# Scattering routed rows to their experts' slots during the layers, and reading them with plain transfers in the expert steps

## The reference, cut to what matters

```python
# attention between 512 tokens x 64 and 32 states x 64, per batch (8) and head (8), both ways
attn_out = concat([softmax(x state^T) state, softmax(state x^T) x], axis=2)   # 544 rows a batch
x = attn_out.transpose(0, 2, 1, 3).reshape(4608, 512)
y = leaky(x @ w_in) @ w_out                     # 512 -> 2048 -> 512, a dense layer
e_idx = argmax(y @ w_gate); gate = softmax(y @ w_gate)[e_idx]
eom = sigmoid(y @ w_output_gate)                # 8 experts, one for each row
for e in range(8):
    out[mask] = gate * eom[:, e] * (relu(y[mask] @ w1[e]) @ w2[e])   # 512 -> 1024 -> 512
```

## Time and profile before

| | us |
|---|---|
| median of 3 runs | 1158.89 (1156.09 to 1159.37) |
| the profiled execution | 1158.76 |
| its span | 1157.0 |
| PE busy in the span | 1114.1 |
| DVE, ACT, POOL busy | 632.6, 405.8, 275.6 |

### The profile page before, as it was taken

The page is one execution under the profiler, slowest core; times in us unless marked ns, Lnnn a source line. Parts: engine busy times, 40 slices in busy tenths (PEclk is TensorE's granted clock), DMA queues, the critical chain, the costliest instruction groups (busy, mean ns, idle before and its releaser), DMA issues.

```text
span 1157.0 us, 18341 instructions
## 1 busy us (share of the span) xinstructions
PE 1114.1 (96%) x6530; PEld 903.9 (78%) x6531; DVE 632.6 (55%) x1421; ACT 405.8 (35%) x754; POOL 275.6 (24%) x337
## 2 busy tenths in 40 slices
PE   5999999999999999999999999999999999888995
PEld 2777777777777777777777888889899989678884
DVE  6684574764854746747554577553433436366342
ACT  4344334434433443344343553321211214244211
POOL 1000001010010010000100203554455365655643
PEclk8999999999999999999999999999999999999998
DMA  9311120120210201200102411761111124443211
GB/s 346 125 45 37 37 78 1 42 73 1 76 40 18 80 19 37 79 1 1 37 1 75 126 38 48 201 195 55 39 48 59 37 56 98 144 105 107 55 39 35
DMA packets 41054, 79.01 MB, mean 68 GB/s; under 512 B 11398, under 2 KB 13190, under 8 KB 40967
## 3 DMA queue, kind: packets, MB, share of 16 engines
q1 hardware_dynamic: 29957, 53.48, 15.2%
q0 software_dynamic: 11040, 24.77, 7.5%
HBM read 60.31 MB, written 20.61 MB: 70 GB/s over the span
## 4 chain that ended last, share of the span: by engine, by line
PE 80%; DVE 6%; issue 4%; DMA 4%; POOL 2%; ACT 1%; POOLq 1%; SPq 0%; DVEq 0%; ACTq 0%
PE bank L529 25%; PE bank L531 24%; PE bank L530 24%; PE bank L562 3%; DMA raw<-w_dram 2%; POOL xq L438 2%; DMA xq<-rows_dram,part_now 2%; PE bank L580 1%; PE bank L596 1%; DVE w_lo L1338 1%; PE bank L604 1%; PE bank L540 1%; PE bank L569 1%; DVE g_buf L1213 0%; DVE o_buf L1600 0%
## 5 line engine op out<-in xcount | busy, mean ns | idle before, releaser
L529 PE MATMUL bank<-wout_lo,gT_hi 128*128 128x512 f32 x544 | 216.0, 397 | 0.0
L531 PE MATMUL bank<-wout_hi,gT_hi 128*128 128x512 f32 x544 | 212.7, 391 | 0.0
L530 PE MATMUL bank<-wout_hi,gT_lo 128*128 128x512 f32 x544 | 212.2, 390 | 0.0
L438 POOL DMA_INDIRECT xq<-rows_dram,part_now x160 | 170.5, 1066 | 69.4 <-issue 54.7
L423 POOL DMA_INDIRECT slots_dram<-tok_i,pos_i x34 | 34.4, 1010 | 616.3 <-DVE pos_i L1313 608.6
L1213 DVE TENSOR_TENSOR g_buf<-g_buf,bank 128x512 f32<-128x512 f32 (+1 forms) x144 | 94.3, 655 | 107.2 <-ACT g_buf L963 106.9
L529 PE MATMUL bank<-xgT_lo,w_hi 128*128 128x256 f32 x512 | 146.3, 286 | 6.0 <-DVE hT_lo L1469 4.7
L530 PE MATMUL bank<-xgT_hi,w_lo 128*128 128x256 f32 x512 | 145.6, 284 | 0.0
L531 PE MATMUL bank<-xgT_hi,w_hi 128*128 128x256 f32 x512 | 145.5, 284 | 0.0
L963 ACT ACTIVATE g_buf<-bank 128x512 f32<-128x512 f32 (+1 forms) x144 | 82.5, 573 | 151.7 <-PE bank L531 150.2
L1217 DVE TENSOR_TENSOR gT_lo<-g_buf,gT_hi 128x512 fp32r<-128x512 f32 (+1 forms) x144 | 95.4, 662 | 72.9 <-ACT gT_hi L969 71.4
(11 more groups left out here) (227 smaller groups left out, 1764.0 us busy)
## 6 DMA issues: line engine op xcount, KB each, us to landing
raw<-w_dram SPq DMA_DIRECT2D x20, 512.0 KB, 8.9
raw<-w_dram SPq DMA_DIRECT2D x10, 1024.0 KB, 14.5
rows_dram<-y_buf SPq DMA_DIRECT2D x8, 1032.0 KB, 4.5
X<-x_in_dram SPq DMA_DIRECT2D x8, 1024.0 KB, 5.5
XT<-xT_in_dram SPq DMA_DIRECT2D x7, 1024.0 KB, 5.7
win<-w_in_dram SPq DMA_DIRECT2D x4, 1024.0 KB, 11.6
y_buf<-w_out_dram POOLq DMA_DIRECT2D x6, 512.0 KB, 7.2
xq<-rows_dram,part_now POOLq DMA_INDIRECT x160
```

Source lines behind the costliest of these rows:

```text
L438: pool.indirect_dma_start(out=xq[:, 4 * u + a, :], out_offset=None, in_=quarters_dram, in_offset=bass.IndirectOffsetOnAxis(ap=part_now[:, ...
L529: pe.matmul(o, l_hi, r_lo, start=first, stop=False)
L530: pe.matmul(o, l_lo, r_hi, start=False, stop=False)
L531: return pe.matmul(o, l_hi, r_hi, start=False, stop=last)
```

## The change

It does this:

- `rows_dram` becomes a table in the order of slots: 8 experts x 4608 slots of 516 floats. `store_rows` goes. In each layer DVE works out a row's slot at f = 12 (`route_rows`), and POOL scatters the 512 rows with four indirect DMAs (`set_rows`) ahead of `set_slots`. `keep_y` waits for them (`rows_set`).
- In layer B the splits of the first expert's first pieces move from f = 8, 10 to 11, 13; gates and ranks from 11 to 8, rows to 9, slots to 10; and the first step's rows are transposed by DVE at f = 14 and split before the layer's last copies.
- A step's rows come with `load_rows`: four plain DMAs of 32 partitions x 8 x 512 bytes and one of 128 x 2 x 8 bytes for the scales, on POOL's queue. `part_row`, `order_rows`, `flip_rows` and the copies of row numbers go.
- Slots behind an expert's last row have to hold finite numbers. SP copies 4.2 MB from `x_in` to slots 256 to 511 of each expert near the start (0.45 MB before, for another purpose), and `fill_tails` writes 256 slots behind each expert's last row from SBUF: eight indirect DMAs of 128 x 4128 bytes, 4.2 MB, and a ninth of at most eight rows. POOL may load the rows of the third and all later steps (those for `turn_quarters(2)` on) only when `filled` shows all nine to have landed.
- `turn_quarters(i + 1)` moves to behind the fifth `h_lo` of a full step and to the front of a half step; PE's first `down` tile waits for each of the last three `h_lo` by itself.
- SP loads the next `w1` as soon as four pieces are split, `w2` after eight.
- The routing of the state rows moves into the first step's `up`.

```diff
-FIRST_PIECE_AT = {0: 2, 3: 3, 8: 0, 10: 1}
+FIRST_PIECE_AT = {0: 2, 3: 3, 11: 0, 13: 1}
-    rows_dram = nc.dram_tensor("rows_dram", (NT, ROW), fp32).ap()
+    rows_dram = nc.dram_tensor("rows_dram", (SLOTS, ROW), fp32).ap()
...
+            sp.dma_start(rows_dram.rearrange("(e s) n -> e s n", e=E)[:, PAIR:2 * PAIR, :],
+                         x_in.rearrange("b s n -> (b s n)")[0:E * PAIR * ROW].rearrange("(e s n) -> e s n", e=E, s=PAIR)).then_inc(slots_clear, 16)
...
-                if b >= 1:
-                    store_rows(b - 1)
...
             sp.wait_ge(ctl_ready, 1)
-            sp.wait_ge(gathered, 64)
+            sp.wait_ge(rows_in, 160)
...
+                    sp.wait_ge(e_lo_done, w1_splits)
+                    load_w1(expert)
                     sp.wait_ge(e_lo_done, splits)
-                    load_expert(expert, between)
+                    load_w2(expert)
-            load_planned(1, between=192)
+            load_planned(1)
...
+            def set_rows(blocks, tiles):
+                pool.wait_ge(slots_clear, 32)
+                pool.wait_ge(row_ready, blocks)
+                for t in range(tiles):
+                    pool.indirect_dma_start(out=rows_dram, out_offset=bass.IndirectOffsetOnAxis(ap=row_i[:, t:t + 1], axis=0),
+                                            in_=y_buf[:, t, :], in_offset=None,
+                                            bounds_check=SLOTS - 1, oob_is_err=False).then_inc(rows_set, 16)
+            def load_rows(col):
+                two = rows_by_tile[bass.ds(col, 2), :, :]
+                for q in range(DC):
+                    pool.dma_start(xq[NS * q:NS * q + NS, :, :],
+                                   two[:, :, QW * q:QW * q + P].rearrange("u (a t) n -> t (u a) n", t=NS)).then_inc(rows_in, 16)
+                pool.dma_start(s_in[:, :, :], two[:, :, P:P + 2].rearrange("u p o -> p u o")).then_inc(rows_in, 16)
+            def fill_tails():
+                pool.wait_ge(rows_set, 64 * B + 32)
+                pool.wait_ge(fill_ready, 1)
+                some_rows = w1_hi[0][:, :, :].bitcast(fp32).rearrange("p k f -> p (k f)")
+                for e in range(E):
+                    pool.indirect_dma_start(out=rows_dram.rearrange("(a two) n -> a (two n)", two=2),
+                                            out_offset=bass.IndirectOffsetOnAxis(ap=fill_i[:, e:e + 1], axis=0),
+                                            in_=some_rows[:, 0:2 * ROW], in_offset=None,
+                                            bounds_check=SLOTS // 2 - 1, oob_is_err=False).then_inc(filled, 16)
...
             with pool.Fori(1, B) as blocks:
+                set_rows(blocks, 4)
                 set_slots(blocks, 4)
+            pool.wait_ge(rows_set, 64 * (B - 1))
+            load_rows(first_col)
+            set_rows(B, 4)
+            set_slots(B, 4)
+            set_rows(B + 1, 2)
+            set_slots(B + 1, 2)
...
+            pool.wait_ge(s_taken, 2)
+            pool.wait_ge(rows_set, 64 * B + 32)
+            load_rows(second_col)
+            fill_tails()
...
+                        pool.wait_ge(filled, 16 * E + 16)
                         pool.wait_ge(s_taken, n)
-                        pool.tensor_copy(part_now[:, :, :], part_row[:, :, bass.ds(col, 2)]).then_inc(rows_copied, 1)
-                        gather_step(n, n)
+                        load_rows(col)
...
-                late = F2 - 1 if tiles == 2 else F2 // 2
+                at_once = 5 if tiles == 2 else F2 // 2
...
+                        elif u == 0 and f >= at_once and tiles == 2:
+                            pe.wait_ge(h_lo_done, F2 * i + f + 1)
...
+            def turn_quarters(i):
+                dve.wait_ge(rows_in, 80 * i + 80)
...
+                    if b == B and f == 14:
+                        dve.wait_ge(y_kept_a, 2 * B)
+                        dve.wait_ge(rows_set, 64 * B)
+                        turn_quarters(0)
...
+            fill_rows()
             plan_order()
...
             plan_steps()
             dve.wait_ge(s_taken, 2)
             dve.tensor_copy(s_now[:, :], s_next[:, :]).then_inc(s_moved, 1)
+            turn_quarters(1)
...
                 if tiles == 2:
-                    for f in range(F2):
+                    for f in range(5):
                         h_lo(i, f)
                     turn_quarters(i + 1)
+                    for f in range(5, F2):
+                        h_lo(i, f)
                 else:
+                    turn_quarters(i + 1)
                     h_lo_turned(i, 0)
-                    turn_quarters(i + 1)
                     h_lo_turned(i, 1)
```

More of the change, by code:

```diff
@@ L425, in set_slots @@
                                             bounds_check=P * COLS - 1, oob_is_err=False).then_inc(slots_set, 16)
[L427 to L440, removed]
@@ L511, in _ @@
             total, after, after2 = load_ctl(pool, 8, MAXP), load_ctl(pool, 25, MAXP + 1), load_ctl(pool, 26, MAXP + 2)
-            all_gathered = load_ctl(pool, 44, 128 * MAXP, 1)
-            gather_step(total, after)
+            all_loaded = load_ctl(pool, 44, 80 * MAXP + 80, 1)
+            pool.wait_ge(filled, 16 * E + 16)
+            pool.wait_ge(s_taken, after)
+            load_rows(first_col)
             next_tokens(after)
@@ L750, in beside_down @@
                     make_v(b, 3)
-                elif f == 11 and r is not None:
+                elif f == (11 if b < B else 8) and r is not None:
                     if b < B:
@@ L791, in _ @@
                 layer(b)
-            def flip_rows(i, halves=(0, 1)):
-                pe.wait_ge(rows_ordered, 2 * i + 2)
-                for n in halves:
-                    for c in (2 * n, 2 * n + 1):
-                        for u in range(2):
-                            o = PAIR * (c % 2) + P * u
-                            last = pe.transpose(t_b[n][:, o:o + P], xr[:, u, c, :], ident)
-                    last.then_inc(t_ready, 1)
             def rows_wait(i, k):
@@ L876, in first_step_and_last_routing @@
                     for k in range(DC):
+                        if f == 0:
+                            rows_wait(0, k)
+                        elif f == 3 and k == 2:
+                            ranks(B, 2, rank_bank=oacc[0])
                         last = product(h_b[f % 4][:, 0:PAIR], w1_hi[0][:, k, fs], w1_lo[0][:, k, fs], xgT_hi[:, k, :], xgT_lo[:, k, :],
@@ L1316, in route_slots @@
                     step(dve.tensor_scalar(tokf[:, 0:T], tokf[:, 0:T], float(S + NS), None, ALU.add))
-                    step.end()
+                step.end()
             w8_row = const[0:1, C_W8:C_W8 + E]
@@ L1346, in states_lo, with rows_lo @@
                 dve.tensor_tensor(sr_lo[:, :, :], sread[:, :, :], sr_hi[:, :, :].bitcast(fp32), ALU.subtract).then_inc(sr_lo_done, 1)
+            def rows_lo(i):
+                for n in range(2):
+                    dve.wait_ge(xg_hi_done, 2 * i + n + 1)
+                    dve.tensor_tensor(xgT_lo[:, 2 * n:2 * n + 2, :], t_b[n][:, :].rearrange("p (c t) -> p c t", c=2),
+                                      xgT_hi[:, 2 * n:2 * n + 2, :].bitcast(fp32), ALU.subtract).then_inc(xg_lo_done, 1)
+            def turn_quarters(i):
+                dve.wait_ge(rows_in, 80 * i + 80)
+                for n in range(2):
+                    dve.transpose(t_b[n][:, :].rearrange("p (k g t) -> p g k t", k=2, t=NS),
+                                  xq[:, :, 2 * NS * n:2 * NS * n + 2 * NS].rearrange("p g (k d) -> p g k d", k=2)).then_inc(t_ready, 1)
+                if not (isinstance(i, int) and i == 0):
+                    dve.wait_ge(s_moved, i)
+                dve.wait_ge(t_ready, 2 * i + 2)
+                dve.tensor_copy(s_next[:, :].rearrange("p (u o) -> p u o", o=1), s_in[:, :, 0:1]).then_inc(s_taken, 2 if isinstance(i, int) and i == 0 else 1)
             def layer(b):
@@ L1419, in _ @@
             dve.memset(ones[:, :], 1.0).then_inc(ones_ready, 1)
-            for q in range(4):
-                dve.memset(quarter[NS * q:NS * q + NS, :], float(q))
             for half in range(2):
```

263 lines of the change are left out of this document (109 added, 154 removed).

## The result

The changed kernel takes 1164.19 us (median of 5 runs, 1162.5 to 1164.8) where the kernel before took 1158.4 beside it: ratio 1.0052, 95% interval 1.0036 to 1.0068. It is slower by 5.8 us; the forecast had 1158.3. The profiled execution took 1162.5 us, its span 1160.9, 3.9 more than before.

The account below looks back on a forecast made before the run. PE bounds the kernel, busy 1114.1 of 1157.0 us. 1158.76 + 9.2 (second step) - 9.7 (half steps and switches) = 1158.3 us; range 1150.5 to 1165.5, likeliest case (gain and loss cancel, 0.38) 1155 to 1162.

Parts of the forecast that it names:

- Layers: Layers before the expert phase: added POOL scatters stay hidden, change taken as 0, upper bound 1 us.
- First step: First expert step: starts at 699.2 without flips and gather wait, second step at 727.0 instead of 729.7; gain not counted.
- Second step: Second expert step: PE idles 11 us at `down`'s sixth block for rows loaded behind the fills; net +9.2 us.
- the clock behind the long wait: Second expert step: slower PE clock after the 11 us idle, costing 1.7 us.
- The starved queue: Second step: weights' burst holds back POOL's fills, landing about 744.5; rival starved to the weights' end: 1163, chance 0.04.
- Half steps and switches: Small experts' five steps: gather waits and late-weight wait go, a split wait of 3.0 comes; 86.6 against 96.3, -9.7 us.
- the 1.6 of clock that was given an even chance: Small experts: slow clock after the 3.0 split wait, 1.6 us at even chance, counted as 0.8.
- the two clock terms named at the start: Small experts before the change: slow PE clock at 1056 to 1059.4 and in step 1005 to 1023, some 3.5 us together.
- the load's "11 us": Half steps: trigger 2.8 us in (5.7 for a new expert), 4.5 issue, 2.5 landing; rows ready before `turn_quarters` at 13.6.
- rival 2: Row loads on POOL's queue no quicker than gathers, 13 us to landing: +6 second step, +2 half steps, 1166; chance 0.22.
- Rival 1: Second step: queues share evenly, fills land at 740.5, PE goes on at 750; 1155, or down to 1150; chance 0.36.
- Rival 3: Second step: wait at `filled` hidden because DVE reaches `turn_quarters(2)` late, after 751; part of rival 1's chance.

Follow-up runs that it names:

- late_w1: Changed kernel with 32 unused bytes ahead of `phase`, but both next-expert weights again wait for all eight splits; 1.0027 of the kernel before.
- after_plus32: Changed kernel with an unused 32-byte tile ahead of `phase`, restoring the earlier SBUF offsets from `XT` on; 0.9906 of the kernel before.
- after_plus32_b: Changed kernel with 32 unused bytes ahead of `phase`, repeated on another chip; 0.9917 of the kernel before.

## Why the prediction was wrong

- **Layers, "I take 0, upper bound 1 us": the step that failed.** Measured +5.4 up to the first step, and +1.5 in the full steps, which were taken as equal ("22.4 before and after"). It looked for waits that the scatters could cause, and PE's waits there came to only 0.2 us more in all (4.0 for 3.8). It did not look at what the diff does to the addresses of tiles it doesn't mention. Shown by moving the tiles alone, in both kernels. Which of the tiles matters, and what in SBUF makes the difference, was not tried.
- **First step.** Forecast 27.8 us from its first product to that of the second step (699.2 to 727.0), measured 28.5. Right within 0.7.
- **Second step.** Right in kind: one wait for the sixth block of `hT_lo`, from the loads behind the fills. Forecast +9.2 up to the third step's end, +9.0 counted from the first step's start, measured +7.0. Counted from that start, the fills landed at 42.8 us (45.3 forecast), PE went on at 52.2 (54.2). So of the idle time, 5.9 for 11.3, 2.0 are rows that came earlier, and 3.4 are no gain but a slower PE: it came to the sixth block at 46.3 (42.9 forecast). The forecast had priced the clock behind the long wait only, at 1.7 us (from rows 4, where it names rows 6), which is about what it cost there. The 2.85 us of idling at the step's start cost clock too, and more, because PE had work through the whole slow stretch:

```profile
732.00:739.50 7.50, 6.62 (x32) 6.62 (x33) 0.88 (x3) 0.77 (x2) 4.04 (x9) 0.54 0.98 325
752.50:760.00 7.50, 3.37 (x9) 2.71 (x10) 5.27 (x10) 4.53 (x6) 3.78 (x5) 0.54 0.40 121
```

  0.54 is the 1.2 GHz level nearly throughout. In the first window PE works at it from 732.88 to 738.9: 28 products of 256 columns at 0.213 us each instead of 0.119, 2.6 us. In the second it works at it only from 756.63 to 759.5: seven products of 512 columns, 1.4 us. The starved queue was wrong: both queues moved. The rule of the Trainium skill ("DMA: Bandwidth & Descriptors", the section on queues, rings and completion order) that a DMA engine goes round robin between its queues fits 737 to 743, 325 of the profile's packets to 300. In 743 to 747 it was 568 to 151; the rows do not tell whether POOL's queue still had work on every engine then, so they neither bear the rule out nor refute it.
- **Half steps and switches.** -9.7 forecast, -8.6 measured, and -9.3 with the layout undone (87.0 for 96.3). The gathers' waits went, one of 2.5 at the weights' split came, and behind it the 1.6 of clock that was given an even chance (24.17 for 22.56, PEclk 0.93). Two small readings were off: the two clock terms named at the start are 1.7 and 2.1, 3.8 and not 3.5, and the terms of the load's "11 us" add up to 9.8, or to 12.7 for a new expert. `late_w1` shows that the early `w1` carries most of the gain: without it 94.6 are left of 96.3.
- **Rivals.** On the chips where the kernel before takes 1158.5, loads took 3.4 us to issue and 4.1 to land, 7.5 and not 13; rival 2 was wrong there, and the slower side came from none of the cases listed. Beside the weights on the slower chips its mechanism is nearer: 11.3 us in `after_plus32` and 11.8 in `after_plus32_b` from the first issue to DVE's start on the rows, over the 10 at which it was to decide. Rival 1 was half right, in its mechanism and not in its time. Rival 3 was wrong: DVE stood 10.84 us waiting for the rows.
- **The sum.** With the layout undone the changed kernel takes 1155.4 us and 0.9968 of the kernel before; 1158.3 was forecast for it, and 1155 to 1162 as the likeliest case's own range. Without that term the forecast would have been 2.9 us too high, and part of that closeness is luck. In its trace the layers take +0.8, first to third step +7.5 (+9.0 forecast), the full steps 0, the small ones -9.3, and the rest to the end -1.8, which the forecast took as 0. Those 1.8 us lie behind the last product of both changed kernels (11.5 us to the end for 13.4 before), and no run says why. The measured 1164.2 lies inside the stated 1150.5 to 1165.5, and that is luck too, since it comes from a term taken as 0.

## What to carry to other kernels

When a change adds or drops a tile, list which other tiles move, and compare the pace of untouched stretches first: equal instruction counts, no gaps and another pace point to the addresses, and one unused tile tells. When a stall goes, read the next instructions of the waiting engine: here rows, weights and fills were each the next to be late, and only moving the bulk write out of the stretch in which weights must arrive won time. A wait on PE can cost more than it shows: behind idles of 2.5, 2.85, 3.0 and 4.8 us the clock cost another 1.6, 2.6, 1.7 and 2.8 here.

## What the hardware showed unexpectedly

- SBUF offsets in steps of 32 bytes change the pace of matmuls with the same instructions: a stretch of the layers takes 18.84, 19.11 and 18.96 us at 0, -32 and -64 bytes, a full expert step 22.42, 22.55 and 21.89, and at -64 in some steps 22.31.
- Chips differ: the kernel before takes 1158, 1167 or 1173 us. The changed kernel with the 32 bytes is at 0.9968 on the first kind and at 0.9906 and 0.9917 on the others, so the change is worth more there. No profile of the kernel before was taken there. Its variant with the tiles 64 bytes lower, on the chip of 1172.9, shows PE pausing 1.6 to 2.5 us in all in the `up` products of three steps, 6 to 10 us behind their start, with nothing shown that it waits for, and a wait of 3.9 us for a gather where the earlier trace rows have 2.2. The variant 32 bytes lower pauses in the same three steps there, so this does not belong to one offset; why is open.
- On the chip of 1172.9 the changed kernel with the 32 bytes had waits of 0.9 us for `scT` in four layers, in both traces taken with it there; on the three other chips no trace with the 32 bytes has one:

```profile
168.93 0.42 DVE L1149 COPY scT<-bank 128x256 f32<-128x256 f32 x1 [2.99 <-remote]
```

  DVE's copy starts 2 us later than its place in the other traces, and nothing that it waits for shows in the trace. POOL issues its row scatters from 163.14 to 168.11 there; that they hold it up was not tried, and stays a guess.
